# Attention, feed-forward and gated convolution on one core: w_out split during the last feed-forward chunk, gate product on VectorE, relu and convolution buffers placed apart from the residual

## The chip, the cores and the metric

The kernel runs on one core of one Trainium2 chip. The metric is the time of one execution on the device in microseconds (us), taken as the median of several runs. Engines are named as in the profile: PE is TensorE (PEld its weight loads), DVE is VectorE, ACT is ScalarE, POOL is GpSimd, SP is SyncE, which only issues transfers. A trailing q ("SPq") is the queue of an engine. "L847" is line 847 of the kernel before.

## The reference, cut to what matters

B = 8 batches, 8 heads, S = 576 positions, head size 64, D = 512 features; everything is float32.

```python
# attention within chunks of 64 positions
attn = softmax(q_c @ k_c.T / sqrt(64)); x = (attn @ v_c), heads merged: [8, 576, 512]
# feed-forward with residual
xn = (x - mean(x)) / sqrt(var(x) + 1e-6) * g_ln
x = x + maximum(xn @ w_ch1, 0) @ w_ch2             # 512 -> 2048 -> 512
# gated convolution
h = maximum(x @ w_in, 0)                           # 512 -> 1024
conv = w[0]*h[s-1] + w[1]*h[s] + w[2]*h[s+1]       # per feature, zero padded at both ends of S
out = (h * sigmoid(conv)) @ w_out                  # 1024 -> 512
```

## The kernel before, in words

All products with weights are computed in float32r with both sides split in a high part and the remainder: hi x hi, hi x lo and lo x hi, three matmuls for one (`split_product`, L375 to L377). So every weight and every moving tile needs two steps: a cast gives the high part (ScalarE, or GpSimd for w_in: L240), and a subtraction gives the low part (GpSimd for weights, L248; VectorE for data).

**Stage one, attention and feed-forward**, runs over NC = 9 chunks of 512 of the 4608 positions. Chunk j does 16 steps f of `up` (w1) and `down` (w2) while the attention of chunk j + 1 is worked in between. At the end of a chunk VectorE adds the residual (`residual`, L780) into `x_cur`, and ScalarE issues the store of it to a scratch tensor in memory (`store_x2`); semaphore `x2_stored` tells that it has landed. The last chunk (8) has no attention beside it.

**Stage two, the gated convolution**, runs over the 8 batches of 576 positions. `load_y` brings a batch's x back into `y_raw` (one buffer), `split_y` makes its high part (ScalarE, L650) and low part (VectorE, L836) in one of two buffers, `y_first` (even batches) and `y_second` (odd). Then for each of GT = 8 feature tiles f:

- TensorE: `gate_up`, 24 matmuls of 288 columns (k = 4, two halves of S, three each) into one of two pairs of PSUM banks. It waits until the relu of the tile two before has emptied its pair.
- ScalarE: `relu` (L656) from PSUM into `h_pad`.
- VectorE: tap 0 (L844, `tensor_scalar`), then taps 1 and 2 (L847), which give `conv`.
- ScalarE: `sigmoid` (L661) on `conv`.
- GpSimd: `gate_step` (L358), the product of `h_pad` and `conv`.
- ScalarE: `gate_hi` (L668), the high part `gh`; VectorE: `gate_lo` (L853), the low part `gl`.

`h_pad` and `conv` have four slots, f modulo 4. The lag is written out by hand: at step f ScalarE does relu(f), gate_hi(f-2), sigmoid(f-1), and VectorE does tap 0, gate_lo(f-3), tap 1, split_y, tap 2, take_tile. `out_tile` (24 matmuls of 512 columns) multiplies 128 positions with w_out, and VectorE's `take_tile` (L860) copies the result out. Nine tiles cover two batches; TensorE does them at the steps in `ODD_TILES` and `EVEN_TILES`, the first of them after the fourth product of batch 1. That one waits for `gl` of all eight tiles of batch 0. Batch 0 has no output tiles beside its eight products, so the first stretch of stage two is twelve products in a row (8 of batch 0, 4 of batch 1) and then an output tile. In batches 2, 4 and 6 ScalarE's gate_hi of tile 0 also waits for output tile 4, which still reads the other batch's columns of `gh`.

**Memory.** Stage two reuses the memory of stage one. Before, `y_second` lay at the start of the late region (`late_at`, with `xnh`, `xnl`, the ring `hh`, `hl`, and `x_cur` in that order in stage one), and `h_pad` and `conv` behind it; `conv` reached into `x_cur`. So ScalarE waits for the store of the last chunk (`act.wait_ge(x2_stored, 16 * NC + 16)`) ahead of batch 0, GpSimd does so ahead of its zeroing of the padding, and w_out is loaded only when all of w1 has been read (`sp.wait_ge(ffn1_done, NC * FT)`). w_out's high parts are then cast by ScalarE inside batch 0, one at each step, and its low parts are made by GpSimd between the gate products.

Each engine takes its own instructions strictly in the written order; semaphores are the only order between engines.

Of the kernel before, what the change touches and what calls it, by code (L numbers as in the profile page):

```python
# [18 lines left out]
F32 = mybir.dt.float32  # L19
# [4 lines left out]
P = 128  # L24
# [38 lines left out]
def build(nc, qv, kk, g_ln, w1, w2, w_in, conv_w, w_out, out):  # L63
# [27 lines left out]
    w1h, w1l, w1_raw = split_weight("w1", [KC, F1])  # L91
# [31 lines left out]

    used[0] = w1h_at
    y_first = place("y_first", [2, KC, S], F32R)
    woh, wol, wo_raw = split_weight("wo", [GT, D])
# [78 lines left out]
    up_done, relu_done, tap_done, sig_done = sem("up_done"), sem("relu_done"), sem("tap_done"), sem("sig_done")  # L205
# [14 lines left out]
    def piece(p):  # L220

        if p < W_IN:
            f = p // 2
            n = f // PER_LOAD * 2 + p % 2
            if p % 2 == 0:
                cols = slice(f * P, (f + 1) * P)
                return n, w1_raw[:, :, cols], w1h[:, :, cols], w1l[:, :, cols]
            return n, w2_raw[:, f, :], w2h[:, f, :], w2l[:, f, :]
# [29 lines left out]
    with block:  # L258
# [3 lines left out]
        def _(sp):  # L262
# [9 lines left out]
            w1_tiles, w2_tiles = w1.rearrange("(k p) n -> p k n", p=P), w2.rearrange("(f p) n -> p f n", p=P)  # L272

            def load_w1(n):

                cols = slice(n * D, (n + 1) * D)
                sp.dma_start(w1_raw[:, :, cols], w1_tiles[:, :, cols]).then_inc(weights_in[2 * n], 16)
# [55 lines left out]
        def _(pool):  # L333
# [15 lines left out]
            pool.wait_ge(x2_stored, 16 * NC + 16)  # L349
# [3 lines left out]

            def gate_step(b, f):

                pool.wait_ge(sig_done, b * GT + f + 1)
                gate = conv[:, f % GSLOTS, :]
                nc.gpsimd.tensor_tensor(gate, h_pad[:, f % GSLOTS, 1:S + 1], gate, ALU.mult).then_inc(gated_done, 1)  # L358

            for f in range(GT):  # L360
                gate_step(0, f)
                split_lo(pool, W_OUT + f)
            with pool.Fori(0, B // 2 - 1) as i:
                for o in range(2):
                    for f in range(GT):
                        gate_step(i * 2 + (o + 1), f)
            for f in range(GT):
                gate_step(B - 1, f)
# [3 lines left out]
        def _(pe):  # L372
# [63 lines left out]
            def up(j, f):  # L436
# [3 lines left out]
                for k in range(KC):  # L440
# [4 lines left out]
                    mm = split_product(ps_hid(f), w1h[:, k, f * P:(f + 1) * P], w1l[:, k, f * P:(f + 1) * P],  # L445
# [105 lines left out]
        def _(act):  # L551
# [44 lines left out]
            def chunk(j, attend, split_weights=False):  # L596
                for f in range(FT):
# [46 lines left out]
            chunk(NC - 1, False)  # L644
# [13 lines left out]

            def sigmoid(b, f):
                act.wait_ge(tap_done, (b * GT + f) * 3 + 3)  # L660
# [26 lines left out]
            act.wait_ge(x2_stored, 16 * NC + 16)  # L687
# [4 lines left out]
            batch(B - 1, 1, split_next=False)  # L692
            gate_hi(B - 1, GT - 2, 1)
            sigmoid(B - 1, GT - 1)
# [223 lines left out]
```

## Time and profile before

| | |
|---|---|
| median of 3 runs | 1373.87 us (1373.07 to 1373.87) |
| the profiled execution | 1372.77 us, span of its instructions 1370.9 us |
| busy: PE, PEld | 1321.6 us (96%), 1121.4 us (82%) |
| busy: DVE, ACT, POOL | 698.8 us (51%), 380.3 us (28%), 177.4 us (13%) |
| chain that ended last | PE 91%, DVE 7%, DMA 1%, ACT 1% |
| granted PE clock, mean | 0.984 of full speed |

Read it from the top: the span is nearly all matmul. The 40 slices of the page show PE at 9 tenths everywhere but in the first two (start of the attention) and in two slices near the 28th, where the page's POOL digit rises and stage two begins. What a change that removes no matmul can move lies there.

### The profile page before, as it was taken

What the parts mean: (1) busy time and instruction counts of PE and PEld (TensorE: products, weight loads), DVE (VectorE), ACT (ScalarE), POOL (GpSimd) and SP (SyncE); (2) the same over time, 40 slices, a digit from 0 to 9 for tenths busy, and PEclk for the clock granted to TensorE, in tenths of its full rate; (3) what the DMA queues carried; (4) which work ended last, traced back from release to release, by engine and by line L of the source; (5) the groups of instructions that cost most, each with busy time, mean ns of one, the idle gap of its engine ahead of it and who ended that gap; (6) DMA issues with size and microseconds to landing.
All of it is one profiled execution on the core that took longest, in us unless ns stands there. A gap on an engine that the chain in (4) does not pass through costs nothing.

```text
span 1370.9 us, 20558 instructions
## 1 busy us (share of the span) xinstructions
PE 1321.6 (96%) x8376; PEld 1121.4 (82%) x8376; DVE 698.8 (51%) x944; ACT 380.3 (28%) x606; POOL 177.4 (13%) x137
## 2 busy tenths in 40 slices
PE   4699999999999999999999999999889999999999
PEld 4478888888888888888888888888779899999997
DVE  4643533534543533634534535213976686676671
ACT  2442322312312312312212313112532333233330
POOL 1442000000000000000000000310632232222230
PEclk8699999999999999999999999999999999999999
DMA  9111011020020110110110100303101101201101
GB/s 338 47 47 47 31 46 46 31 69 23 31 69 23 46 53 23 54 46 23 54 54 14 54 23 0 127 0 126 37 8 59 49 32 57 73 15 50 39 16 54
DMA packets 30636, 69.62 MB, mean 51 GB/s; under 512 B 2448, under 2 KB 2448, under 8 KB 30608
## 3 DMA queue, kind: packets, MB, share of 16 engines
q1 hardware_dynamic: 25856, 59.79, 12.4%
q10 hardware_dynamic: 4752, 9.44, 1.8%
q8 instruction: 20, 0.33, 0.1%
q14 instruction: 8, 0.07, 0.0%
HBM read 50.35 MB, written 18.87 MB: 50 GB/s over the span
## 4 chain that ended last, share of the span: by engine, by line
PE 91%; DVE 7%; DMA 1%; ACT 1%; issue 1%; SPq 0%; DVEq 0%
PE ps L375 28%; PE ps L377 27%; PE ps L376 27%; PE ps L421 3%; PE ps L394 3%; DVE conv L847 2%; PE ps L406 1%; DVE prob L726 1%; DVE row_sum L720 1%; DVE y_second L836 1%; DVE conv L844 0%; DMA k_sb<-in_kk 0%; DVE hl L773 0%; DVE xc L762 0%; DMA x_scratch<-x_cur 0%
## 5 line engine op out<-in xcount | busy, mean ns | idle before, releaser
L773 DVE SCALAR_TENSOR_TENSOR hl<-ps,hh 128x512 fp32r<-128x512 f32 x144 | 99.5, 691 | 359.0 <-ACT hh L580 359.0
L375 PE MATMUL ps<-xnh,w1h 128*128 128x512 f32 x576 | 229.2, 398 | 4.4 <-DVE xnl L768 4.4
L375 PE MATMUL ps<-hh,w2h 128*128 128x512 f32 x576 | 227.4, 395 | 0.0
L377 PE MATMUL ps<-xnh,w1l 128*128 128x512 f32 x576 | 225.3, 391 | 0.0
L376 PE MATMUL ps<-xnl,w1h 128*128 128x512 f32 x576 | 225.2, 391 | 0.0
L377 PE MATMUL ps<-hh,w2l 128*128 128x512 f32 x576 | 224.5, 390 | 0.0
L376 PE MATMUL ps<-hl,w2h 128*128 128x512 f32 x576 | 224.1, 389 | 0.0
L580 ACT ACTIVATE hh<-ps 128x512 fp32r<-128x512 f32 x144 | 86.0, 597 | 452.4 <-PE ps L377 452.4
L847 DVE SCALAR_TENSOR_TENSOR conv<-h_pad,cw_sb,conv 128x576 f32<-128x576 f32 x128 | 144.1, 1125 | 1.4
L358 POOL TENSOR_TENSOR conv<-h_pad,conv 128x576 f32<-128x576 f32 x64 | 105.3, 1645 | 263.2 <-ACT conv L661 263.2
L375 PEld LDWEIGHTS ps<-xnh,w1h 128*128 128x128 f32 x576 | 108.5, 188 | 28.8 <-DVE xnl L768 4.6
L377 PEld LDWEIGHTS ps<-xnh,w1l 128*128 128x128 f32 x576 | 108.5, 188 | 22.9
L377 PEld LDWEIGHTS ps<-hh,w2l 128*128 128x128 f32 x576 | 108.1, 188 | 23.0
L376 PEld LDWEIGHTS ps<-xnl,w1h 128*128 128x128 f32 x576 | 108.4, 188 | 21.5
L376 PEld LDWEIGHTS ps<-hl,w2h 128*128 128x128 f32 x576 | 108.3, 188 | 21.6
L375 PEld LDWEIGHTS ps<-hh,w2h 128*128 128x128 f32 x576 | 108.2, 188 | 21.4
L375 PE MATMUL ps<-woh,gh 128*128 128x512 f32 x288 | 113.7, 395 | 4.7 <-DVE gl L853 4.7
L377 PE MATMUL ps<-woh,gl 128*128 128x512 f32 x288 | 113.3, 393 | 0.0
L376 PE MATMUL ps<-wol,gh 128*128 128x512 f32 x288 | 113.2, 393 | 0.0
L240 POOL CAST wih<-wi_raw 128x512 fp32r<-128x512 f32 x8 | 4.9, 613 | 756.6 <-DMA wi_raw<-in_w_in 756.6
L656 ACT ACTIVATE h_pad<-ps 128x576 f32<-128x576 f32 x64 | 41.6, 650 | 192.2 <-PE ps L377 181.2
L844 DVE TENSOR_SCALAR conv<-h_pad,cw_sb 128x576 f32<-128x576 f32 x64 | 35.5, 555 | 106.7 <-ACT h_pad L656 106.7
(97 smaller groups left out, 1945.9 us busy)
## 6 DMA issues: line engine op xcount, KB each, us to landing
qv_sb<-in_qv SPq DMA_DIRECT2D x34, 512.0 KB, 3.3
x_scratch<-x_cur ACTq DMA_DIRECT2D x9, 1024.0 KB, 4.3
y_raw<-x_scratch SPq DMA_DIRECT2D x8, 1152.0 KB, 5.7
out<-o_sb SPq DMA_DIRECT2D x36, 256.0 KB, 2.0
k_sb<-in_kk SPq DMA_DIRECT2D x34, 256.0 KB, 3.5
w_raw<-in_w SPq DMA_DIRECT2D x8, 1024.0 KB, 13.6
wi_raw<-in_w_in SPq DMA_DIRECT2D x1, 2048.0 KB, 7.5
wo_raw<-in_w_out SPq DMA_DIRECT2D x1, 2048.0 KB, 8.4
```

Of the source, the lines that this page charges most:

```text
L358: nc.gpsimd.tensor_tensor(gate, h_pad[:, f % GSLOTS, 1:S + 1], gate, ALU.mult).then_inc(gated_done, 1)
L375: nc.tensor.matmul(o, wh, xh, start=first, stop=False)
L376: nc.tensor.matmul(o, wh, xl, start=False, stop=False)
L377: return nc.tensor.matmul(o, wl, xh, start=False, stop=last)
L394: mm = nc.tensor.matmul(ps_score(c, gl_)[h, cols], qv_of[h, cols], k_of[h, cols], start=True, stop=True)
L406: mm = nc.tensor.transpose(ps_att[:, t * P:(t + 1) * P], prob_at_group(c, gl_)[:, t * P:(t + 1) * P], ident[:, :])
L421: mm = nc.tensor.matmul(ps_val(c, gl_)[u, to], qv_of[u, (8 + p) * QC:(9 + p) * QC], probT[u, p * QC:(p + 1) * QC], start=True, stop=True)
L580: nc.scalar.activation(hh[:, f % RING, :], ps_hid(f), ACT.Relu).then_inc(hh_done, 1)
L656: nc.scalar.activation(h_pad[:, f % GSLOTS, 1:S + 1].rearrange("p (s n) -> p s n", s=2), ps_gate(f), ACT.Relu).then_inc(relu_done, 1)
L773: nc.vector.scalar_tensor_tensor(hl[:, f % RING, :], ps_hid(f), 0.0, hh[:, f % RING, :].bitcast(F32), ALU.max, ALU.subtract).then_inc(hl_d ...
L844: nc.vector.tensor_scalar(c, h, cw_sb[:, f, 0:1], None, ALU.mult).then_inc(tap_done, 1)
L847: nc.vector.scalar_tensor_tensor(c, h, cw_sb[:, f, t:t + 1], c, ALU.mult, ALU.add).then_inc(tap_done, 1)
```

## The change

- w1 is held, and passed in from the host, as [feature tile][k][column] in place of [k][all columns]; each f then frees one contiguous tile of `w1h` and one of `w1l` when its last `up` is done. A load of w1 moves 8 KB in one piece for each partition.
- The high part of w_out lies at the start of `w1h`, then `y_first`, then w_out raw and low in `w1l`. The load of w_out waits for the ninth `up` of the last chunk. ScalarE casts two pieces of it at each of steps 12 to 15 of that chunk (`split_out`), and GpSimd makes the low parts as they come, ahead of zeroing the padding.
- `load_y(1)` is issued ahead of the wait for the last store, behind the load of w_out.
- `h_pad` and `conv` change places with `y_second` in the late region. What waits for the last store is now ScalarE's first split into `y_second`, at step 2 of batch 0; GpSimd zeroes the padding once the last `up` is done.
- In batch 0 tap 0 is done by ScalarE (`first_tap`), behind the relu of the same tile. ScalarE's order at a step becomes relu, (first_tap), sigmoid(f-1), gate_hi(f-2).
- The gate product moves from GpSimd to VectorE, between tap 1 and tap 2. VectorE's order at a step: tap 0 (not in batch 0), gate_lo(f-3), tap 1, gate_step(f-1), tap 2, split_y, take_tile.

```diff
-    w1h, w1l, w1_raw = split_weight("w1", [KC, F1])
+    w1h, w1l, w1_raw = split_weight("w1", [FT, KC * P])
...
     used[0] = w1h_at
+    woh = place("woh", [GT, D], F32R)
     y_first = place("y_first", [2, KC, S], F32R)
-    woh, wol, wo_raw = split_weight("wo", [GT, D])
+    wo_raw = at("wo_raw", [GT, D], F32, used[0])
+    wol = place("wol", [GT, D], F32R)
+    WO_FREE = GT + 1
...
     used[0] = late_at
-    y_second = place("y_second", [2, KC, S], F32R)
     GSLOTS = 4
     h_pad = place("h_pad", [GSLOTS, S + 2])
     conv = place("conv", [GSLOTS, S])
+    y_second = place("y_second", [2, KC, S], F32R)
...
-            sp.wait_ge(ffn1_done, NC * FT)
+            sp.wait_ge(ffn1_done, (NC - 1) * FT + WO_FREE)
             sp.dma_start(wo_raw[:, :, :], w_out.rearrange("(f p) n -> p f n", p=P)).then_inc(weights_in[-1], 16)
+            load_y(1)
             sp.wait_ge(x2_stored, 16 * NC + 16)
-            load_y(1)
...
-            pool.wait_ge(x2_stored, 16 * NC + 16)
+            for p in range(W_OUT, W_END):
+                split_lo(pool, p)
+            pool.wait_ge(ffn1_done, NC * FT)
...
+                    if split_out and f >= FT - GT // 2:
+                        for p in range(2):
+                            split_hi(act, nc.scalar.copy, W_OUT + (f - (FT - GT // 2)) * 2 + p)
...
+            def first_tap(f):
+                act.wait_ge(relu_done, f + 1)
+                need(act, gl_done, f - GSLOTS + 1)
+                nc.scalar.mul(conv[:, f % GSLOTS, :], h_pad[:, f % GSLOTS, 0:S], cw_sb[:, f, 0:1]).then_inc(tap0_done, 1)
...
                 for f in range(GT):
                     relu(b, f)
+                    if first:
+                        first_tap(f)
+                    if f >= 1 or not first:
+                        sigmoid(*before(b, f, 1))
                     if f >= 2 or not first:
                         gate_hi(*before(b, f, 2), odd if f >= 2 else 1 - odd, tiles_done if f == 2 else None)
-                    if f >= 1 or not first:
-                        sigmoid(*before(b, f, 1))
-                    if first:
-                        split_hi(act, nc.scalar.copy, W_OUT + f)
+                    if first and f == split_from:
+                        act.wait_ge(x2_stored, 16 * NC + 16)
...
-            act.wait_ge(x2_stored, 16 * NC + 16)
+            act.wait_ge(small_in, 32)
+            act.wait_ge(pad_done, 2 * GSLOTS)
             batch(0, 0, first=True)
...
+            def gate_step(b, f):
+                dve.wait_ge(sig_done, b * GT + f + 1)
+                gate = conv[:, f % GSLOTS, :]
+                nc.vector.tensor_tensor(gate, h_pad[:, f % GSLOTS, 1:S + 1], gate, ALU.mult).then_inc(gated_done, 1)
...
                 for f in range(GT):
-                    tap(b, f, 0)
+                    if not first:
+                        tap(b, f, 0)
                     if f >= 3 or not first:
                         gate_lo(*before(b, f, 3), odd if f >= 3 else 1 - odd)
                     tap(b, f, 1)
+                    if f >= 1 or not first:
+                        gate_step(*before(b, f, 1))
+                    tap(b, f, 2)
                     if split_next and 0 <= f - split_from < KC:
                         split_y(b + 1, 1 - odd, f - split_from)
-                    tap(b, f, 2)
```

## Rows read from the trace of the kernel before

**Rows 1.** Waits of PE in stage two (900 to 1371 us): total us, times, longest
```profile
PE ps L375 <- ACT h_pad L656: 6.1, 6, 2.0
PE ps L375 <- DVE gl L853: 4.7, 1, 4.7
```
**Rows 2.** Timeline of PE: start us, duration us, line, output<-inputs, [idle before <-releaser]
```profile
948.84 0.29 PE L375 MATMUL ps<-y_first,wih 128*128 128x288 f32 x1
...
955.10 0.29 PE L377 MATMUL ps<-y_first,wil 128*128 128x288 f32 x1
955.39 0.40 PE L375 MATMUL ps<-y_first,wih 128*128 128x288 f32 x1
...
1001.58 0.79 PE L375 MATMUL ps<-woh,gh 128*128 128x512 f32 x1 [4.75 <-DVE gl L853]
...
1009.07 0.29 PE L375 MATMUL ps<-y_second,wih 128*128 128x288 f32 x1
```
**Rows 3.** Timeline of DVE, the last two output tiles
```profile
1362.31 0.69 DVE L860 COPY o_sb<-ps 128x512 f32<-128x512 f32 x1 [4.75 <-PE ps L377]
1367.75 0.69 DVE L860 COPY o_sb<-ps 128x512 f32<-128x512 f32 x1 [4.75 <-PE ps L377]
```
**Rows 4.** Stretch, its us, busy PE PEld DVE ACT POOL, granted clock, DMA share, GB/s
```profile
1000.00:1005.00 5.00, 3.42 (x8) 2.75 (x9) 4.96 (x7) 2.58 (x4) 1.52 (x2) 0.50 0.00 0
```
**Rows 5.** Chain of work that ended last, around the first relu: start us, us, what
```profile
949.77 4.90 DMA x_scratch<-x_cur
954.69 0.66 ACT h_pad L656
```
**Rows 6.** Timeline of POOL, as in Rows 2
```profile
880.92 1.30 POOL L248 TENSOR_TENSOR wil<-wi_raw,wih 128x512 fp32r<-128x512 f32 x1
...
983.57 1.37 POOL L358 TENSOR_TENSOR conv<-h_pad,conv 128x576 f32<-128x576 f32 x1 [2.14 <-ACT conv L661]
984.90 1.80 POOL L248 TENSOR_TENSOR wol<-wo_raw,woh 128x512 fp32r<-128x512 f32 x1
```
**Rows 7.** Timeline of DVE, in batch 0 and later beside an idle POOL
```profile
983.80 3.52 DVE L847 SCALAR_TENSOR_TENSOR conv<-h_pad,cw_sb,conv 128x576 f32<-128x576 f32 x2
...
1069.48 0.52 DVE L844 TENSOR_SCALAR conv<-h_pad,cw_sb 128x576 f32<-128x576 f32 x1 [1.62 <-ACT h_pad L656]
1069.92 0.75 DVE L853 TENSOR_TENSOR gl<-conv,gh 128x576 fp32r<-128x576 f32 x1
1070.59 0.81 DVE L847 SCALAR_TENSOR_TENSOR conv<-h_pad,cw_sb,conv 128x576 f32<-128x576 f32 x1
1071.32 1.98 DVE L836 TENSOR_TENSOR y_second<-y_raw,y_second 128x576 fp32r<-128x576 f32 x1
```
**Rows 8.** Timeline of ACT, end of the last chunk and stage two
```profile
941.38 2.39 ACT L650 CAST y_first<-y_raw 128x576 fp32r<-128x576 f32 x4
...
956.42 1.28 ACT L661 ACT_TABLE_LOAD   x1
...
1012.46 0.65 ACT L656 ACTIVATE h_pad<-ps 128x576 f32<-128x576 f32 x1 [7.69 <-PE ps L377]
1013.01 0.67 ACT L668 CAST gh<-conv 128x576 fp32r<-128x576 f32 x1
1013.57 0.69 ACT L661 ACTIVATE conv<-conv 128x576 f32<-128x576 f32 x1
1014.16 0.67 ACT L650 CAST y_first<-y_raw 128x576 fp32r<-128x576 f32 x1
...
1056.92 0.67 ACT L668 CAST gh<-conv 128x576 fp32r<-128x576 f32 x1 [8.09 <-PE ps L377]
```
**Rows 9.** Line L773 in 878 to 897 us: duration ns min/median/max, starts
```profile
L773 DVE SCALAR_TENSOR_TENSOR hl<-ps,hh x3: 690/692/693, 881.7 to 892.6; 128x512 fp32r<-128x512 f32 x3
```
**Rows 10.** Timeline of PE at the start of the kernel
```profile
8.18 1.97 PE L394 MATMUL ps<-k_sb,qv_sb 64*64 64x64 f32 x32 [1.43 <-DMA k_sb<-in_kk]
```
**Rows 11.** DMA issues on the page: count, KB each, us from issue to landing
```profile
wo_raw<-in_w_out SPq DMA_DIRECT2D x1, 2048.0 KB, 8.4
```

More of the change, by code:

```diff
@@ L121, in build @@
     assert used[0] <= nc.sbuf_usable_end
+    W1_TILE = 4 * KC * P
     used[0] = w1h_at
+    woh = place("woh", [GT, D], F32R)
     y_first = place("y_first", [2, KC, S], F32R)
-    woh, wol, wo_raw = split_weight("wo", [GT, D])
+    assert used[0] <= w1h_at + (FT + 1) * W1_TILE
+    wo_raw = at("wo_raw", [GT, D], F32, used[0])
+    wol = place("wol", [GT, D], F32R)
+    WO_FREE = GT + 1
+    assert used[0] <= w1h_at + (FT + WO_FREE) * W1_TILE
     OST = 3
@@ L204, in build @@
     y_in, yh_done, yl_done, pad_done = sem("y_in"), sem("yh_done"), sem("yl_done"), sem("pad_done")
-    up_done, relu_done, tap_done, sig_done = sem("up_done"), sem("relu_done"), sem("tap_done"), sem("sig_done")
+    up_done, relu_done, sig_done = sem("up_done"), sem("relu_done"), sem("sig_done")
+    tap0_done, tap_done = sem("tap0_done"), sem("tap_done")
     gated_done, gh_done, gl_done = sem("gated_done"), sem("gh_done"), sem("gl_done")
@@ L225, in piece @@
             if p % 2 == 0:
[L226 to L227 removed]
+                return n, w1_raw[:, f, :], w1h[:, f, :], w1l[:, f, :]
             return n, w2_raw[:, f, :], w2h[:, f, :], w2l[:, f, :]
@@ L270, in load_group @@
                 sp.dma_start(k_to, kk[g]).then_inc(landed, 16)
-            w1_tiles, w2_tiles = w1.rearrange("(k p) n -> p k n", p=P), w2.rearrange("(f p) n -> p f n", p=P)
+            w2_tiles = w2.rearrange("(f p) n -> p f n", p=P)
             def load_w1(n):
-                cols = slice(n * D, (n + 1) * D)
-                sp.dma_start(w1_raw[:, :, cols], w1_tiles[:, :, cols]).then_inc(weights_in[2 * n], 16)
+                tiles = slice(n * PER_LOAD, (n + 1) * PER_LOAD)
+                sp.dma_start(w1_raw[:, tiles, :], w1[:, tiles, :]).then_inc(weights_in[2 * n], 16)
             def load_w2(n):
@@ L352, in _ @@
                 nc.gpsimd.memset(h_pad[:, s, S + 1:S + 2], 0.0).then_inc(pad_done, 1)
[L354 to L368, printed above, removed]
         @block.tensor
@@ L594, in hi_of_sum, with chunk @@
                 nc.scalar.copy(ln_hi[:, :], ln_sum[:, :]).then_inc(lnh_done, 1)
-            def chunk(j, attend, split_weights=False):
+            def chunk(j, attend, split_weights=False, split_out=False):
                 for f in range(FT):
@@ L643, in _ @@
                 chunk(j, True)
-            chunk(NC - 1, False)
+            chunk(NC - 1, False, split_out=True)
             def split_y(b, odd, k):
@@ L692, in _ @@
             batch(B - 1, 1, split_next=False)
+            sigmoid(B - 1, GT - 1)
             gate_hi(B - 1, GT - 2, 1)
-            sigmoid(B - 1, GT - 1)
             gate_hi(B - 1, GT - 1, 1)
@@ L843, in tap @@
                     dve.wait_ge(relu_done, n + 1)
-                    nc.vector.tensor_scalar(c, h, cw_sb[:, f, 0:1], None, ALU.mult).then_inc(tap_done, 1)
+                    nc.vector.tensor_scalar(c, h, cw_sb[:, f, 0:1], None, ALU.mult).then_inc(tap0_done, 1)
                 else:
-                    dve.wait_ge(tap_done, n * 3 + t)
+                    if t == 1:
+                        dve.wait_ge(tap0_done, n + 1)
+                    else:
+                        dve.wait_ge(tap_done, n * 2 + 1)
                     nc.vector.scalar_tensor_tensor(c, h, cw_sb[:, f, t:t + 1], c, ALU.mult,
                                                    ALU.add).then_inc(tap_done, 1)
+            def gate_step(b, f):
+                dve.wait_ge(sig_done, b * GT + f + 1)
+                gate = conv[:, f % GSLOTS, :]
+                nc.vector.tensor_tensor(gate, h_pad[:, f % GSLOTS, 1:S + 1], gate, ALU.mult).then_inc(gated_done, 1)
             def gate_lo(b, f, odd):
@@ L885, in _ @@
             batch(B - 1, 1, B // 2 - 1, LAST_TILES, split_next=False)
+            gate_step(B - 1, GT - 1)
             for f in range(GT - 3, GT):
```

6 lines of the change are left out of this document (3 added, 3 removed).

## The prediction

> **What bounds the kernel now.** I read the page first: matmuls fill 96% of the span, and the change removes none of them, so only time in which TensorE stands still or runs slow can be won. Next the waits of TensorE over stage two: they come to 10.8 us and all lie in its first stretch, six waits for a relu and one of 4.7 us for the last low part of the gate [rows 1]. Then TensorE's timeline gives the true loss, which is larger than the waits. The first product of batch 0 starts at 948.84, and its 48th matmul (the end of the second product) at 955.10, so one matmul takes (955.10 - 948.84) / 47 = 0.133 us and a product of 24 takes 3.20 [rows 2]. An output tile takes 1367.75 - 1362.31 = 5.44 [rows 3]. Twelve products and one tile make 12 x 3.20 + 5.44 = 43.84 us, yet the batch goes on after the tile only at 1009.07: 60.23 us [rows 2]. **The loss is 16.39 us.** What is not in the wait rows is mainly clock: the tile, begun after 4.75 us of idleness, takes 1009.07 - 1001.58 = 7.49 us, 2.05 too many [rows 2], and the granted clock beside it is 0.50, that is 1.2 in place of 2.4 GHz [rows 4]. I book the lower clock as a consequence of the idling: it goes if the waits go.
>
> Who causes the waits? The chain shows the store of the last chunk (949.77, 4.90 us) and then the first relu at 954.69 [rows 5]; the product it reads was ready at 948.84 + 3.20 = 952.04. From there VectorE never stops, and its operations are long beside GpSimd: two taps take 3.52 us while GpSimd's product and w_out subtraction run [rows 6, 7], against 0.81 for one tap when GpSimd is idle [rows 7]. So batch 0 is paced by VectorE, slowed by GpSimd.
>
> **The change part by part.** All times below are on the clock of the profiled execution of before.
>
> *Relu off the store.* ScalarE starts a relu 0.19 us after TensorE is through with the product: the first one behind the tile ended at 1009.07 + 3.20 = 1012.27, and the relu starts at 1012.46 [rows 2, 8]. So relu(0) starts at 952.23 in place of 954.69 and TensorE's first wait (its third product began at 955.39, not 955.24) goes. The wait for the store now stands ahead of the first cast into y_second, step 2 of ScalarE, which I put at about 961.5. The store has landed by 949.77 + 4.90 = 954.7 [rows 5], so the wait costs nothing; behind it would be relu(3), due at 961.83. The second load of y is issued earlier too, and nobody waits for it before that cast.
>
> *w_out into the last chunk.* The load takes 8.4 us [rows 11]; the ninth `up` of the chunk ends 7 steps of 5.44 = 38 us ahead of the last relu (just before the casts at 941.38 [rows 8]) and the first cast comes 3 steps = 16 us ahead of it, so the data are there with 13 us to spare. ScalarE's eight casts, about 0.6 us each (four casts of y take 2.39 [rows 8]), lie two by two behind a relu, where it has only the relu to do in each 5.44: nothing on the path, but the last two push the casts of y from 941.38 to 942.4. GpSimd's eight subtractions, 1.30 each beside an idle VectorE [rows 6], run beside VectorE's low parts L773, which read PSUM and took 0.69 while GpSimd was splitting w_in [rows 9]: no cost. The last two GpSimd subtractions overlap the split of y(0), which reads SBUF twice. Bounds for its four low parts: 0.67 us apart (as L853, from 1069.92 to 1070.59) or 1.98 each, as beside GpSimd [rows 7]. Started at 943.1 they end at 946 or 951. I take two slow and two fast, 948.4. TensorE needs the first by 948.84 and the last k by 951.24: no wait at either end. The residual add then ends by 951 (two slow) or 954 (four slow) and with it the store's issue, which ScalarE has ahead of relu(0): 0 or about 1.5 us of delay to the relu. I take 0. What goes from batch 0: ScalarE's eight casts and all of GpSimd's work.
>
> *Gate product on VectorE, tap 0 of batch 0 on ScalarE.* With GpSimd idle I take VectorE's start-to-start times from rows: tap 0 0.43 (1069.48 to 1069.92), a two-input product or subtraction 0.67, a later tap 0.73 (1070.59 to 1071.32) [rows 7]. No row shows the gate product on VectorE. Bounds: 0.67, the subtraction of the same shape, and 1.37, what GpSimd took [rows 6]; I take 0.67, since it is the same operation kind, size and type on the same engine. ScalarE's first_tap has no row either: bounds 0.65 and 0.75 (the fastest other ScalarE pass of this size, and one tenth more); I take 0.67 [rows 8]. Step sums for VectorE: with gate_lo, tap 1, gate, tap 2 and a split of y, 3.47; without the split 2.80; in batch 1 with tap 0, 3.23.
>
> Now the chain. Relu(1) starts at 955.43, its tap 0 at 956.15; then the sigmoid table is loaded, 1.28 us [rows 8], as before behind relu(1): sigmoid(0) runs from 958.1 to 958.8. Gate(0) starts at 958.85, tap 2 of tile 1 at 959.52 and ends at 960.33; sigmoid(1) to 961.1, gate(1) 961.15, tap 2 of tile 2 961.82, and the first split of y(1) 962.55. From its end at 963.22 VectorE has no wait left: its input is always there, because ScalarE's step (relu 0.55 and the wait for its end 0.12, tap 0.6, sigmoid 0.59, gate_hi 0.57, cast 0.57 [rows 8]: 3.0) is shorter than 3.20. So steps 3, 4, 5 take 3 x 3.47, steps 6 and 7 2 x 2.80, steps 0 and 1 of batch 1 2 x 3.23, and then tap 0 and the subtraction of gate tile 7, 0.43 + 0.75: 963.22 + 10.41 + 5.60 + 6.46 + 1.18 = **986.9**. TensorE, unhindered, has done its twelve products at 948.84 + 38.40 = **987.24**. So the output tile finds its gl ready with 0.3 us to spare. In between, product n needs the relu of n - 2, which ends 0.85 us after that product against 3.20 to spare; the latest, relu(3) at about 962.8, is 2 us early.
>
> The Trainium skill, page ScalarE: Activation LUTs, in its section on what ACT_TABLE_LOAD costs, says that each per-partition pointer operand adds about 93 ns to an ACTIVATE. No row of the trace isolates that. By it first_tap would be some 0.76 us, two of them would shift the chain by up to 0.2, and the margin would be 0.1.
>
> With a margin of 0.3 I leave 0.2 us for a short wait. **Gain 16.39 - 0.2 = 16.2 us.**
>
> *Later batches.* The gate product adds 0.67 to VectorE's step, which then holds 3.23 against 3.20 of a product. The place that could wait is the tile after four products in a row: VectorE starts 0.85 after the first product, needs 3.23 + 3.23 + 1.18 and is done at 8.5; TensorE comes at 4 x 3.20 - 3.20 = 9.6. Slack 1.1 us, and each output tile gives VectorE 5.44 us in between. Where ScalarE stands 8.09 us before gate_hi for output tile 4 [rows 8], the sigmoid of the tile before is now ahead of that wait, so the gate product does not hang on it. Cost 0. At the very end the last sigmoid, gate product and two halves lie beside output tiles 2 and 3, 10.9 us: 0.
>
> *Layout of w1.* The matmuls read the same 128 columns at another address: 0. Its loads run behind the second attention group's, for which TensorE waits 1.43 us [rows 10]. Larger pieces can shift the start by anything from that gain to the same loss; the first 20 us wait otherwise on the softmax chain. I take 0.
>
> **Sum.** The span goes from 1370.9 to 1354.7, the profiled execution from 1372.77 to 1356.6. Three runs had their median at 1373.87, 1.10 above the profiled execution, so the median becomes 1373.87 - 16.2 = **1357.7 us**.
>
> **The rivals.**
>
> *VectorE becomes the bound of batch 0.* There are 35 VectorE operations between 963.22 and the gate's last low part, and the margin is 0.3. If each takes 0.1 us more than my rows (a handover from ScalarE, a dearer gate product), TensorE waits 3.2 us at the first output tile, and up to 2.05 us of lower clock may come on top, as before: 1360.7 to 1362.7, say 1361.5. For it: VectorE would run without a pause. Against it: the rows beside an idle GpSimd repeat to 0.01 us. Chance 0.13.
>
> *The start shifts* by over 1 us with the w1 loads, or the granted clock is released at another moment: 1356.3 or 1359.1. Chance 0.04, both signs.
>
> *The gate product serialises the later batches, and the kernel is slower.* Gate(f-1) on VectorE waits for sigmoid(f-1), which stands behind relu(f) on ScalarE, and tap 2 of f is queued behind it. VectorE gets there 0.43 + 0.67 + 0.73 = 1.83 us after the relu, ScalarE needs 0.7. If that handover took so long that each of the twelve operations ahead of a tile were 0.35 us later, 4.2 less the slack of 1.1 would be waited at each of seven places: 21.7 us, giving 1379.4. It decides from 1.1 us on, and turns the sign from 1.1 + 16.2 / 7 = 3.4 us. Nothing in the rows speaks for it. Chance 0.02.
>
> *It doesn't do what it says*: something else of the last chunk holds relu(0) to about 955 and the gain is only paid back at the tile, within 0.2% (about what a measurement of this kernel can tell from no change). Chance 0.01.
>
> **How the numbers follow.** The forecast has 0.80, with its own range 1356.6 to 1359.3. The range to hold 8 in 10 reaches below for the start (1356.0) and above to the VectorE rival's middle (1361.5). Faster by over 0.2% (under 1371.1): 0.80 + 0.13 + 0.04 = 0.97; same 0.01; slower 0.02.
>
> **What would show it.** Right: relu(0) about 3.4 us after the first y_first matmul; no GpSimd row after the padding; two taps at 0.81 each; the first woh matmul 38.4 us after the first y_first one, clock 1.00 there; no wait of TensorE in stage two. Wrong in my margin: one wait for gl at that tile and a clock under 1. Wrong altogether: waits for gl at the tile 0 or 4 of later batches, or a wait for the low part of y ahead of batch 0.

## The result, and the profile after

| | before | after |
|---|---|---|
| median of the first comparison (4 runs each) | 1373.87 us (1373.07 to 1374.12) | 1355.74 us (1354.98 to 1356.89) |
| again, beside the experiments (15 and 4 runs) | 1373.89 us (1373.04 to 1375.14) | 1356.33 us (1354.92 to 1357.50) |
| ratio, 95% interval | | 0.987 (0.9853 to 0.9887); again 0.9868 (0.9853 to 0.9883) |
| profiled execution, its span | 1372.77, 1370.9 us | 1356.89, 1355.1 us |

The kernel is 1.3% faster: 18.1 us by the first medians, 17.6 by the second. The forecast was 1357.7 (1356.0 to 1361.5), a gain of 16.2. The low end of that range was just missed by the first median's 1355.74 and held by the second's 1356.33; both lie below the 1356.6 at which the prediction's own range for its main case began.

The page of the kernel after (its lines of busy time, slices of PE, DVE and POOL, and the granted clock):

```profile
PE 1315.3 (97%) x8376; PEld 1118.1 (83%) x8376; DVE 663.1 (49%) x1000; ACT 386.3 (29%) x614; POOL 68.6 (5%) x73
...
PE   4699999999999999999999999999999999999999
...
DVE  4643633533533633534543543412876566566661
POOL 1442000000000000000000000043000000000000
PEclk9699999999999999999999999999999999999999
```

VectorE does 56 operations more (x1000 against x944 in the kernel before: 64 gate products come, 8 taps go) and is busy for less: 663.1 us against 698.8. The 64 products (48.0 us) have not lengthened it, because its other work has become short: taps 1 and 2 went from 144.1 to 103.7 us for the same 128, the low parts of y from 48.2 to 25.0 us for the same 32. GpSimd has nothing to do after the 28th slice.

TensorE has no wait left in stage two. Its timeline after, at the places of [rows 2]:

```profile
950.26 0.29 PE L367 MATMUL ps<-y_first,wih 128*128 128x288 f32 x1
...
988.66 0.39 PE L367 MATMUL ps<-woh,gh 128*128 128x512 f32 x1
...
994.12 0.30 PE L367 MATMUL ps<-y_second,wih 128*128 128x288 f32 x1
```

Twelve products take 988.66 - 950.26 = 38.40 us and the output tile behind them 5.46. Before, it was 52.74 and 7.49 [rows 2]. The stretches over the same two parts (us, busy PE, PEld, DVE, ACT, POOL, granted clock, DMA share, GB/s) answer to [rows 4]: the clock is 1.00 in both.

```profile
950.26:988.66 38.40, 38.40 (x290) 38.39 (x289) 31.64 (x47) 28.11 (x43) 0.00 (x0) 1.00 0.25 89
988.66:994.12 5.46, 5.46 (x27) 4.50 (x26) 4.98 (x8) 1.90 (x3) 0.00 (x0) 1.00 0.00 0
```

ScalarE's timeline after, for [rows 5, 8]: the first relu comes 3.48 us behind the first y_first matmul and not behind the store, which was issued at 951.18.

```profile
951.18 0.58 ACTq L582 DMA_DIRECT2D x_scratch<-x_cur  x1
953.74 0.65 ACT L651 ACTIVATE h_pad<-ps 128x576 f32<-128x576 f32 x1 [7.51 <-PE ps L369]
954.42 0.78 ACT L657 ACTIVATE conv<-h_pad,cw_sb 128x576 f32<-128x576 f32 x1
...
958.34 1.28 ACT L661 ACT_TABLE_LOAD   x1
959.63 0.69 ACT L661 ACTIVATE conv<-conv 128x576 f32<-128x576 f32 x1
```

VectorE's timeline after, for [rows 7]: the split of y(0) and the residual, the gate product (L859) between two taps (L853), and at the end the low part of gate tile 7, for which the output tile waited before.

```profile
944.53 3.97 DVE L839 TENSOR_TENSOR y_first<-y_raw,y_first 128x576 fp32r<-128x576 f32 x4 [0.91 <-ACT y_first L645]
948.49 2.66 DVE L783 TENSOR_TENSOR x_cur<-ps,x_cur 128x512 f32<-128x512 f32 x4
...
965.34 0.81 DVE L853 SCALAR_TENSOR_TENSOR conv<-h_pad,cw_sb,conv 128x576 f32<-128x576 f32 x1
966.07 0.75 DVE L859 TENSOR_TENSOR conv<-h_pad,conv 128x576 f32<-128x576 f32 x1
966.74 0.81 DVE L853 SCALAR_TENSOR_TENSOR conv<-h_pad,cw_sb,conv 128x576 f32<-128x576 f32 x1
...
987.54 0.75 DVE L864 TENSOR_TENSOR gl<-conv,gh 128x576 fp32r<-128x576 f32 x1
```

The gate product starts 0.73 behind a tap and takes 0.67 to the next: what was assumed. Tile 7's low part ends at 988.29, 0.37 us ahead of TensorE at 988.66.

**Where the time came from**, trace against trace, counted from the first y_first matmul to the end of the span (422.06 us before, 404.84 after): 52.74 - 38.40 = 14.34 in the products, 7.49 - 5.46 = 2.03 in the first output tile, 0.85 in all later batches together; 17.22 in all. What lies ahead of the first y_first matmul took 1.42 us more in this pair of executions (948.84 and 950.26), which is why the two spans differ by only 15.8. That part varies from execution to execution, as the next section shows.

### The profile page after: what moved, and what is told of

Same layout as the page of the kernel before. It is cut to its first block, busy times and chain, and to the rows that moved or that the text cites. A ratio compares the mean times of both kernels' runs of the same rounds, so it can differ in the third digit from the quotient of the medians.

```text
span 1355.1 us, 20456 instructions
## 1 busy us (share of the span) xinstructions
PE 1315.3 (97%) x8376; PEld 1118.1 (83%) x8376; DVE 663.1 (49%) x1000; ACT 386.3 (29%) x614; POOL 68.6 (5%) x73
## 4 chain that ended last, share of the span: by engine, by line
PE 95%; DVE 4%; ACT 1%; DMA 0%; issue 0%; SPq 0%; DVEq 0%
PE ps L367 29%; PE ps L369 29%; PE ps L368 29%; PE ps L413 3%; PE ps L386 3%; PE ps L398 1%; DVE prob L729 1%; DVE row_sum L723 1%; DMA k_sb<-in_kk 0%; DVE hl L776 0%; DVE xc L765 0%; ACT hh L572 0%; PE ps L426 0%; PE ps L422 0%; PE ps L421 0%; DVE ln_sum L762 0%
## 5 line engine op out<-in xcount | busy, mean ns | idle before, releaser
L853 DVE SCALAR_TENSOR_TENSOR conv<-h_pad,cw_sb,conv 128x576 f32<-128x576 f32 x128 | 103.7, 811 | 5.6 <-ACT conv L657 5.5
L847 DVE TENSOR_SCALAR conv<-h_pad,cw_sb 128x576 f32<-128x576 f32 x56 | 28.9, 516 | 119.0 <-ACT h_pad L651 119.0
L369 PE MATMUL ps<-y_second,wil 128*128 128x288 f32 x256 | 76.1, 297 | 0.0
L367 PE MATMUL ps<-y_first,wih 128*128 128x288 f32 x256 | 75.7, 296 | 0.0
```

The lines of the kernel that those rows point to most:

```text
L367: nc.tensor.matmul(o, wh, xh, start=first, stop=False)
L369: return nc.tensor.matmul(o, wl, xh, start=False, stop=last)
L847: nc.vector.tensor_scalar(c, h, cw_sb[:, f, 0:1], None, ALU.mult).then_inc(tap0_done, 1)
L853: nc.vector.scalar_tensor_tensor(c, h, cw_sb[:, f, t:t + 1], c, ALU.mult, ALU.add).then_inc(tap_done, 1)
```

## The experiments

In the table the "products" are the time from the first y_first matmul to the first output tile, "rest" is from the end of that tile to the end of the span; both and the tile are from each kernel's one profiled execution. The medians are beside runs of the kernel before on the same chip, which had 1373.89, 1374.30 and 1374.05.

| kernel | median us | products | first tile | rest |
|---|---|---|---|---|
| before | 1373.89 | 52.74 | 7.49 | 361.83 |
| after, again | 1356.33 | 38.40 | 5.46 | 360.96 |
| layout_only | 1373.94 | 52.72 | 7.60 | 361.97 |
| groups_first | 1356.28 | 38.39 | 5.46 | 360.94 |
| store_first | 1357.81 | 39.36 | 5.59 | 360.97 |
| tap0_vector | 1358.03 | 39.86 | 5.57 | 360.97 |
| store_and_tap0 | 1360.27 | 41.42 | 7.22 | 360.98 |
| gate_pool | 1361.20 | 41.81 | 7.19 | 362.42 |
| wout_late | 1364.02 | 45.50 | 5.57 | 361.01 |
| gpsimd_both | 1370.89 | 49.99 | 6.94 | 362.42 |
| lo_twice | 1361.97 | 40.09 | 5.57 | 364.19 |
| normalise_first | 1350.40 | 38.40 | 5.46 | 360.99 |

**The changed kernel again (after_again).**

> The changed kernel once more, as the yardstick of this set. Against the kernel before the trace of the changed kernel shows 17.2 us gained from the first y_first matmul on and 1.4 us lost before it. Theory A (the start varies from execution to execution by the moment at which TensorE's clock rises): this run lands between 1354 and 1357, and its first y_first matmul moves by up to 1.4 us against the 950.26 of the first trace, while the 38.4 us from there to the first output tile stay. Theory B (the w1 layout costs 1.4 us at the start, always): the first y_first matmul is again at 950.3.

Measured 1356.33 (1354.92 to 1357.50), the first y_first matmul at 950.78. That value alone does not decide between the two theories. The traces of the runs below do: with the same w1 layout and the same loads at the start, the first y_first matmul comes anywhere from 948.98 (gate_pool) to 951.35 (lo_twice), which a constant cost does not give, while the time from it to the end of the span repeats to 0.06 us in the four traces whose stage two is that of the changed kernel (404.79 to 404.85). So the scatter sits ahead of stage two. What sets it (theory A named the moment at which the clock rises) is not shown.

**The w1 layout alone (layout_only).**

```diff
--- before
-    w1h, w1l, w1_raw = split_weight("w1", [KC, F1])
+    w1h, w1l, w1_raw = split_weight("w1", [FT, KC * P])
...
-                sp.dma_start(w1_raw[:, :, cols], w1_tiles[:, :, cols]).then_inc(weights_in[2 * n], 16)
+                sp.dma_start(w1_raw[:, tiles, :], w1[:, tiles, :]).then_inc(weights_in[2 * n], 16)
...
```

> The kernel before with the new layout and host order of w1 alone, so that its loads move 8 KB in one piece. Theory A (the layout does nothing): 1373.9 within 1 us, first y_first matmul at 948.8 to 949.8. Theory B (larger pieces of w1 hold up the attention groups): the wait for the second group is 1.7 us in place of 1.43, and the start 0.4 to 1.4 us later: 1374.3 to 1375.3. Theory C (larger pieces land sooner and help): 1372.5 to 1373.

Measured 1373.94 over 11 runs against 1373.89 over 15: ratio 0.9999 (0.999 to 1.0008). The layout does nothing that these runs can tell. Its profiled execution had the first y_first matmul at 950.71, outside the 948.8 to 949.8 of theory A and as late as the changed kernel's, yet its median is that of before; so the 1.42 us by which the two first traces differ at the start is no steady cost of the layout. What differs there from execution to execution can be read at the start of stage one. TensorE's timeline has the second attention group and the first w1 matmul, in the kernel before (the second group is [rows 10]) and in layout_only:

```profile
59.87 0.56 PE L375 MATMUL ps<-xnh,w1h 128*128 128x512 f32 x1 [4.40 <-DVE xnl L768]
```
```profile
8.35 1.97 PE L393 MATMUL ps<-k_sb,qv_sb 64*64 64x64 f32 x32 [1.53 <-DMA k_sb<-in_kk]
...
61.29 0.80 PE L374 MATMUL ps<-xnh,w1h 128*128 128x512 f32 x1 [5.70 <-DVE xnl L767]
```

In layout_only stage one begins 1.42 us later, and its first matmul is 0.80 long and not 0.56: the granted clock over the first 2 us is 0.50 against 0.58. Of the twelve traces with this layout eleven began like that and one (gate_pool) with 0.52; of the kernel before there is one trace, and with 1372.77 us it is quicker than all but one of the 37 runs of before beside the experiments. So the first comparison of two traces set a quick start against an ordinary one. The interval leaves room for a cost of the layout of up to 1.1 us or a gain of up to 1.4; the second groups' waits of 1.47 to 2.21 us in its traces (with the order of loads as before) against 1.43 would fit a small cost, but one trace of before can't show it.

**The first weights behind all attention groups (groups_first).**

```diff
--- after
                 load_group(0, gl_)
-                if gl_ == 1:
-                    load_w1(0)
-                    load_w2(0)
+            load_w1(0)
+            load_w2(0)
```

> The changed kernel with the first loads of w1 and w2 behind all four attention groups in place of behind the second. If transfers of one queue are served strictly in order, the second group's wait (1.68 us) does not move and the time is that of the changed kernel, 1355.7 within 1. If w1 and w2 compete with the second group, that wait shrinks by up to 1.7 us and so does the time: 1354.

The second group's wait did shrink, from 1.43 to 2.21 us in all other traces to 0.99 in this one (timeline of TensorE):

```profile
7.78 1.97 PE L385 MATMUL ps<-k_sb,qv_sb 64*64 64x64 f32 x32 [0.99 <-DMA k_sb<-in_kk]
```

The time did not move: 1356.28 (1355.32 to 1356.71) against 1356.33. So this one trace points to loads queued later taking something from an earlier one: its wait is 0.44 us under the shortest of the others. Nothing of it is seen in the median; with a scatter of over 2 us ahead of stage two, half a microsecond can't be told. Inconclusive on the time.

**The relu behind the store again (store_first).**

```diff
--- after
+            act.wait_ge(x2_stored, 16 * NC + 16)
             batch(0, 0, first=True)
...
-                    if first and f == split_from:
-                        act.wait_ge(x2_stored, 16 * NC + 16)
```

> The changed kernel with ScalarE's wait for the last store put back ahead of batch 0 (and not at step 2). In the changed kernel's trace the store is issued at 951.18, so with 4.9 us it lands at 956.1; relu(0) then starts 2.4 us later than its 953.74. My theory (VectorE paces batch 0 without a pause and has 0.37 us in hand at the first output tile): TensorE waits 2.0 us in the stretch, plus 0 to 2 us of lower clock: 1357.7 to 1359.8. Rival (the store was what held batch 0, GpSimd's work was hidden): most of the 16 us comes back, 1368 or more. Rival (nothing is on the path here): 1355.7.

Measured 1357.81: +1.5 us by the median, +0.96 in the products and +0.13 in the tile by the trace. The time is at the low end of what was expected, and the wait is half of the 2.0 us that I had put. Relu(0) came 3.1 us later (956.80 with the same start of y_first within 0.02), but only 1 us of it arrived at the output tile. The reason is in the first steps: in the changed kernel VectorE stands still between them for the next relu, tap 0 and the sigmoid, and those idle times swallow 1.8 us of the delay: the first gate product on VectorE comes only 1.3 us later than in the changed kernel (961.65 against 960.35), and the reserve takes 0.37 of that. The rival in which the store was the cause of the 16 us is out.

**Tap 0 of batch 0 back on VectorE (tap0_vector).**

```diff
--- after
-                    if first:
-                        first_tap(f)
...
-                    if not first:
-                        tap(b, f, 0)
+                    tap(b, f, 0)
```

> The changed kernel with tap 0 of batch 0 on VectorE again. My theory (VectorE is the bound of the twelve products, 0.37 us in hand): 8 x 0.43 = 3.4 us more on VectorE, less the 0.37 and less the 0.2 us or so that the first tile gets sooner: TensorE waits 2.9 us, mostly at the first output tile, plus 0 to 2 us of lower clock: 1358.6 to 1360.7. Rival (the chain is paced by the handovers between ScalarE and VectorE, not by VectorE's work): tap 0 is taken off ScalarE's path, so no change, 1355.7.

Measured 1358.03: +1.46 in the products, one wait of 1.3 us for gl. Half of what was expected. The sign is that of my theory (VectorE is the bound), the size is not. VectorE's timeline of this kernel ends the low part of tile 7 at

```profile
988.86 0.74 DVE L862 TENSOR_TENSOR gl<-conv,gh 128x576 fp32r<-128x576 f32 x1
```

989.60, that is 39.80 us after its first y_first matmul (949.80) against 38.03 in the changed kernel: 1.77 later, of which the reserve of 0.37 takes its part. The working: the first low part of y(1) starts 13.36 us after the first y_first matmul (963.16) against 13.74 in the changed kernel (964.00), so the first three steps became 0.38 shorter, their taps falling into VectorE's idle times and being done sooner than ScalarE does them (0.52 long against 0.78). The five taps of tiles 3 to 7 add 5 x 0.43 = 2.15, and 2.15 - 0.38 = 1.77. What I had wrong was to charge all eight.

**Both of these undone (store_and_tap0).**

> The changed kernel with the two other parts undone: the wait for the store back ahead of batch 0, and tap 0 of batch 0 on VectorE. Alone they lengthened the twelve products by 0.96 and 1.46 us. Theory (one VectorE chain with 0.37 us in hand): 0.96 + 1.46 + 0.37 = 2.8 us more, 41.2 us for the products, and 1359 to 1360.5, a little more if the clock falls. Together with the run that puts GpSimd's jobs back it accounts for the kernel before: 52.74 = 38.4 + 2.8 + 11.5. Rival (what is left is a matter of GpSimd alone): 1356.

The edit is that of the last two together. Measured 1360.27, products 41.42, that is +3.02: 0.96 + 1.46 + 0.37 = 2.79 was expected. The two share the one reserve of 0.37 us. The tile took 7.22 in place of 5.46, at a lower granted clock (stretches of this kernel, columns as above):

```profile
985.00:990.00 5.00, 4.30 (x33) 4.06 (x31) 5.00 (x9) 2.15 (x5) 0.00 (x0) 1.00 0.00 0
990.00:995.00 5.00, 3.90 (x12) 3.12 (x13) 5.00 (x9) 3.03 (x5) 0.00 (x0) 0.74 0.00 0
```

TensorE had waited 0.8 us at 957.04 and then 1.8 us just ahead of the tile. In tap0_vector it had waited 1.3 us just ahead and in wout_late 2.3, and their tiles took 5.57 at a granted clock of 1.00.

**The gate product back on GpSimd (gate_pool).**

```diff
--- after
+            for f in range(GT):                       # GpSimd, batch 0; the later batches likewise
+                gate_step(0, f)
...
-                    if f >= 1 or not first:           # VectorE
-                        gate_step(*before(b, f, 1))
```

> The changed kernel with the gate product of all batches on GpSimd again; all else stays. My theory (a GpSimd product keeps VectorE off its second input for its whole length): VectorE saves 0.67 per step and loses about 1.4, so 0.7 to 1.1 us a step over 11 steps less 0.37: 7 to 12 us waited in the first stretch, some of it at lower clock, 1363 to 1368; taps of 1.65 to 2 us in the trace. Rival (GpSimd's product is hidden, what slowed batch 0 was its w_out work): VectorE is shorter by 0.67 per step and the time stays 1355.7.

Measured 1361.20: +3.41 in the products, +1.73 in the tile (a granted clock of 0.76 over it, after a wait of 3.2 us) and +1.46 in later batches. The rival is out: VectorE has one operation less a step and is later. The size was too high. VectorE's two taps beside GpSimd's product, from its timeline:

```profile
974.90 0.75 DVE L854 TENSOR_TENSOR y_second<-y_raw,y_second 128x576 fp32r<-128x576 f32 x1
975.57 0.75 DVE L874 TENSOR_TENSOR gl<-conv,gh 128x576 fp32r<-128x576 f32 x1
976.24 2.62 DVE L868 SCALAR_TENSOR_TENSOR conv<-h_pad,cw_sb,conv 128x576 f32<-128x576 f32 x2
```

The pair takes 2.62 where two free taps take 0.73 + 0.81 = 1.54: 1.08 lost for 0.67 saved, 0.4 a step and not the 0.7 to 1.1 I had put. Over the whole kernel VectorE is busy for 690.6 us with 64 operations less than in the changed kernel, which has 663.1.

**w_out split in batch 0 again (wout_late).**

```diff
--- after
-            for p in range(W_OUT, W_END):             # GpSimd
-                split_lo(pool, p)
             pool.wait_ge(ffn1_done, NC * FT)
...
+            for p in range(W_OUT, W_END):             # behind the zeroing of the padding
+                split_lo(pool, p)
...
-            chunk(NC - 1, False, split_out=True)
+            chunk(NC - 1, False)
...
+                    if first:                         # ScalarE, batch 0
+                        split_hi(act, nc.scalar.copy, W_OUT + f)
```

> The changed kernel with w_out split in batch 0 as before (ScalarE one cast per step, GpSimd's eight subtractions there), though it is loaded early; the gate product stays on VectorE. My theory: each subtraction takes 1.3 to 1.8 us of VectorE's second input, about 1.1 us lost to VectorE each, eight times 1.1 less 0.37 = 8.4 us waited plus 0 to 2 of lower clock: 1364 to 1366. ScalarE's step gets 0.5 us longer, 3.5 us against the 3.2 of a product: by itself 8 x 0.3 = 2.4. Rival (only the gate product did harm): 1355.7 to 1358.

Measured 1364.02, at the low end of what was expected; +7.10 in the products, where I had put 8.4. TensorE's waits in the stretch name two engines:

```profile
PE ps L367 <- ACT h_pad L651: 3.5, 4, 1.2
PE ps L367 <- DVE gl L866: 2.3, 1, 2.3
```

and the two timelines show one subtraction of w_out and the VectorE operation that ran into it, behind the one place at which VectorE stood idle after its first gate product:

```profile
968.12 1.74 POOL L254 TENSOR_TENSOR wol<-wo_raw,woh 128x512 fp32r<-128x512 f32 x1 [2.09 <-ACT woh L246]
```
```profile
965.05 1.58 DVE L841 TENSOR_TENSOR y_second<-y_raw,y_second 128x576 fp32r<-128x576 f32 x1 [0.18 <-ACT y_second L645]
...
968.63 1.84 DVE L855 SCALAR_TENSOR_TENSOR conv<-h_pad,cw_sb,conv 128x576 f32<-128x576 f32 x1
```

VectorE's timeline settles which of the two counts. The low part of tile 7 comes 7.41 us later than in the changed kernel, counted from the first y_first matmul. Seven VectorE operations ran into a subtraction, and each put the one behind it off by 0.84 to 1.08 us, 7.14 in all; only 0.26 is waiting for ScalarE, whose step the casts had lengthened. So of GpSimd's two jobs in batch 0 it was the w_out split that cost more, 7.1 against 3.4 us, because it held VectorE up without taking anything off it.

**Both GpSimd jobs back (gpsimd_both).**

> The changed kernel with both of GpSimd's jobs put back into batch 0: the gate product of all batches, and the w_out split (one cast of ScalarE and one subtraction a step); the relu stays off the store and tap 0 of batch 0 stays on ScalarE. Alone, the one lengthened the twelve products of 38.4 us by 3.4 and the other by 7.1. Theory (GpSimd's reads of SBUF hold VectorE up for their length, so the jobs add where VectorE is already the bound, and the first to come pays for the room of 0.37 us for both): 10.5 to 12 us more, 49 to 50.5 us, and with the lower clock in the tile (about 2) and 1.5 in later batches 1370 to 1372. Rival (they hide behind each other): 45.5 to 47 us, 1364 to 1367.

The edit is that of the last two, GpSimd's subtraction now between its products as in the kernel before. Measured 1370.89, products 49.99: +11.59, where the two alone made 3.41 + 7.10. They add, and a little more: with the reserve of 0.37 us, which each alone could use and both together only once, they make 10.88. The 0.7 us above that I can't place. VectorE's timeline has the pair of taps at

```profile
976.73 3.73 DVE L869 SCALAR_TENSOR_TENSOR conv<-h_pad,cw_sb,conv 128x576 f32<-128x576 f32 x2
```

0.2 longer than the 3.52 of [rows 7]. With store_and_tap0 nearly the whole kernel before is accounted for. The end of the low part of tile 7, counted from the first y_first matmul, has no reserve in it: 38.03 in the changed kernel, 11.91 later in gpsimd_both, 3.33 later in store_and_tap0, which makes 53.27, against 52.68 in the kernel before. The 0.6 us between the two is what the parts that no run undid alone (the order of sigmoid and gate_hi on ScalarE, the split of y behind tap 2, the earlier load of y(1)) and interactions can have made.

**The slack of VectorE in later batches (lo_twice).**

```diff
--- after
                     if not first:
+                        lo_early(*before(b, f, 3), odd if f >= 3 else 1 - odd)   # the same subtraction, once more
                         tap(b, f, 0)
+                        dve.wait_ge(early_lo, (b - 1) * GT + f + 1)
```

> The changed kernel in which, from batch 1 on, VectorE makes each low part of the gate twice, the first one ahead of tap 0: 0.67 us more per step. It prices the slack of VectorE in later batches: in the trace the low part of tile 7 is ready 0.99 us ahead of the output tile that needs it. Two of the three extra operations fall between relu(0) and that moment, 1.34 us: 0.35 to 0.45 us of wait at each of seven places, and 3 x 0.67 - 0.37 = 1.6 us at the first output tile: 4.1 to 4.8 in all, plus 0 to 2 of lower clock, 1359.8 to 1362.5. If the later batches had far more room, only the 1.6: 1357.3. If they had none (the rival in which the gate product serialises them), 7 x 1.34 + 1.6: 1366 or more.

Measured 1361.97: +1.69 in the products, +0.11 in the tile, +3.23 in the rest. The places in the rest are six and not seven: one tile after four products in a row in each of batches 2 to 7, the one of batch 1 being the first tile itself. So it is 0.54 at each. The profile shows them as six waits (the idle times leave out the gap that the modelled end of the last matmul covers):

```profile
PE ps L368 <- DVE gl L865: 1.6, 6, 0.3
```

The later batches have about the room that the prediction gave them, 1.1 us by its sum, 0.99 in the trace, and no more than that: of the 1.34 us put in, 0.54 came out, so 0.80 was free. About 0.1 of what is missing is the tile itself, 5.57 long in place of 5.46 or 5.49.

**One reordering in stage one (normalise_first).**

```diff
--- after
+                    if attend and f == 1:
+                        normalise(j + 1, SCORE_AT[f])
                     relu_lo(j, f)
                     if attend:
-                        if f in SCORE_AT:
+                        if f in SCORE_AT and f > 1:
                             normalise(j + 1, SCORE_AT[f])
```

> The changed kernel with one reordering in stage one: at step 1 of each chunk VectorE normalises the attention group of the next chunk ahead of the low part of the relu, which it otherwise waits for. In the changed kernel's trace TensorE waits eight times for the normalised group, 4.8 us shown, some 6 with the gap that the modelled ends hide. Theory: VectorE is idle for 2 us at that place, the eight waits go and nothing else is late: 1356.3 - 6 = 1350.3, within 1.5. Rival (the low part of the relu comes late and the third up waits for it): 1355 or more.

Measured 1350.40 (1349.56 to 1352.27), ratio to the kernel before 0.9827 (0.9814 to 0.9841): 6 us under the changed kernel (on another chip than after_again; the kernel before had 1374.05 on it and 1373.89 on the other). In the changed kernel TensorE's waits in stage one read

```profile
PE ps L367 <- DVE xnl L771: 5.3, 1, 5.3
PE ps L398 <- DVE prob L729: 4.8, 8, 1.6
```

and the second line is gone in this one, with one wait of 0.9 us for another input in its place. With the tail at no wait at all, the next thing to gain was eight small waits at the start of the chunks, and VectorE was idle just ahead of them. It is the best of the kernels here.

## Why the prediction was right, and where its sizes were off

- **The ceiling of the gain, 16.39 us, was too low by 0.8.** Its two parts were right: 14.34 in the products and 2.03 in the tile came back in full, 16.37. What I left out is the rest, 361.83 us before and 360.98 after. The step that failed is "Cost 0" for the later batches: I asked what the gate product adds to VectorE and not what GpSimd's going takes off it. Before, VectorE had the low part of tile 7 ready only at the moment at which the output tile behind four products wanted it, 0.08 to 0.16 us ahead of it; after, 0.98 to 1.07. VectorE and TensorE in the kernel before:

```profile
1050.27 0.75 DVE L853 TENSOR_TENSOR gl<-conv,gh 128x576 fp32r<-128x576 f32 x1
```
```profile
1051.15 0.49 PE L375 MATMUL ps<-woh,gh 128*128 128x512 f32 x1
```

  and in the kernel after:

```profile
1034.32 0.76 DVE L864 TENSOR_TENSOR gl<-conv,gh 128x576 fp32r<-128x576 f32 x1
```
```profile
1036.07 0.40 PE L367 MATMUL ps<-woh,gh 128*128 128x512 f32 x1
```

  The first matmul of the tile is 0.49 long in place of 0.40, and that tile with its start took 0.13 more than its like after. There are six such tiles: three took 0.13 more, the three between them 0.05 to 0.08, together 0.6 of the 0.85. Other tiles of odd batches went from 5.49 to 5.46, some ten of them, which makes the rest and for which I have no cause. gate_pool confirms the sign: with only the product back on GpSimd the rest is 1.46 longer than after. That it is more than 0.85 stays open (its order on ScalarE is not that of before).
- **The chain of VectorE** was predicted to end its low part at 986.9, 38.06 us after the first y_first matmul; it ended 38.03 after it (988.29). The reserve was put at 0.3 and is 0.37; the 0.2 us that I left for a short wait was not needed. The sum holds from its start: the first gate product came 0.08 later after the first y_first matmul than in it, the first split of y(1) 0.03 later.
- **first_tap** was taken at 0.67 and is 0.78, above the upper of its two bounds. A cast of the same size is 0.66 to 0.67 on this engine, so it takes 0.11 us more; no run took its per-partition operand away, so that this is the reason is not shown. The page ScalarE: Activation LUTs of the Trainium skill, in its section on what ACT_TABLE_LOAD costs, gives 93 ns for such an operand, and by it the estimate was 0.76: here the page was nearer than my choice. The shift of the chain by up to 0.2 that I had worked out from it did not come: 0.08 us were left of it at the first gate product and 0.03 at the first split of y.
- **w_out in the last chunk**: no cost. y(0) was split in 3.97 us for four, between my bounds; one of its four low parts was long (1.84, the others 0.75), where I had put two. Its end was at 948.50 against 948.4 on a clock 1.42 us earlier, a good microsecond sooner than I had put it; TensorE's first product did not wait. The residual ended at 951.15 and the store was issued at 951.18, 2.6 us ahead of relu(0).
- **The cause I named for the pace of batch 0**, VectorE slowed by GpSimd, is borne out by gate_pool, wout_late and gpsimd_both: 11.6 of the 14.3 us. The Trainium skill's page SBUF — State Buffer, in its section on who interferes with whom, says that VectorE and GpSimd share a port pair as an exclusive lock, that a VectorE operation with two SBUF inputs contends with a GpSimd one that reads SBUF, and that one with at most one SBUF input, outside the modes that use both pairs, does not. The rows agree for taps 1 and 2, products and subtractions (a tap 0.81 alone, 1.84 beside a w_out subtraction), and for its other half: L773, with one input in PSUM, kept its 0.69 beside GpSimd [rows 9]. It kept it in the changed kernel too (0.68 to 0.69 for all 144), so w_out could be split beside it at no cost. One tensor input in SBUF is no safe mark: tap 0, which has no more, took 1.56 beside a w_out subtraction in the kernel before, against 0.52.

```profile
960.79 1.56 DVE L844 TENSOR_SCALAR conv<-h_pad,cw_sb 128x576 f32<-128x576 f32 x1
```

- **The median.** I moved the median by the gain of the trace, from 1373.87, and the reference was sound (1373.89 and 1374.05 over 15 runs each). 17.2 us of trace gain in the place of 16.4 would have given 1356.7. The measured 1355.74 and 1356.33 lie within the scatter of that, which sits ahead of stage two. They lie next to the 1356.3 that I gave to an earlier start, but that is chance: the start did not come sooner in the two traces of this kernel (950.26 and 950.78 against 948.84).
- **The rivals.** VectorE as the bound of batch 0, with 0.13, did not come, but it was near: 35 operations and a reserve of 0.37 us mean that some 0.01 us more in each would have used it up; lo_twice and tap0_vector show the wait appear as soon as the reserve is used. The serialising gate product did not come: the one wait of a product for a sigmoid in the stretch is 1.2 us, at the table load.

## What to carry to other kernels

Where a trace shows VectorE's operations on SBUF longer beside GpSimd's, the two should not both stream SBUF operands in a stretch in which one of them is the bound. Giving the slower engine's work to the busier one made that one less busy (690.6 us in gate_pool, 663.1 with the product on VectorE), since a product on GpSimd held VectorE up for longer (1.08) than the product takes on VectorE (0.67). When work has to be prepared on the second engine, put it beside operations of the first that read PSUM (here 0.69 with and without GpSimd). And count what a removed neighbour gives back everywhere it was, not only at the place that waits.

## What the runs showed of the hardware that I had not expected

- An ACTIVATE of 128x576 float32 from SBUF with a per-partition scale takes 0.78 us; the sigmoid of the same size, without one, takes 0.67 to 0.69.
- The granted clock after a wait ahead of the first tile. Where the last wait was 1.3 us (tap0_vector), 1.5 (lo_twice) or 2.3 (wout_late), the tile took 5.57 at a clock of 1.00. Where it was 1.8 (store_and_tap0), 3.2 (gate_pool), 4.75 (before) or 4.9 (gpsimd_both), it took 6.9 to 7.5 at 0.73 to 0.79. Earlier waits don't sort them either: wout_late had four more in the stretch, 3.5 us in all, gate_pool none. So a wait of about two microseconds may cost its own length, or nearly double that; which of the two was not foreseeable from its length.
- Ten traces with the same loads at the start of the program reach stage two at 948.98 to 951.35 us, while the 400 us from there to the end repeat to 0.06 us in the four traces with the same stage two.
